# Attention and two expert stages on one core: queries turned once, fillers for TensorE, and value products of two key blocks at a time

## The reference, cut to what matters

```python
# attention: B=4, H=8, S=1152, D=64
q_pool = q.reshape(B, H, S // 2, 2, D).mean(axis=3)      # 576 queries a head
scores = q_pool @ k.T / sqrt(D)
attn = exp(scores - max) ; attn /= attn.sum + 1e-9
x = attn @ v                                             # 2304 rows of 512
# SoLU: x 2304x512, w_in 512x1024, w_out 1024x512
h = x @ w_in ; solu = h * softmax(h)
ln = (solu - mean) / sqrt(var + 1e-6) * g_ln ; x = ln @ w_out
# experts: 8, each 512x1024 and 1024x512, the chosen one times its gate
```

## Time and profile before

| | us |
|---|---|
| median of 3 executions | 1127.13 (1125.83 to 1127.24) |
| the profiled execution | 1129.12 |
| its span, first to last instruction | 1127.4 |
| TensorE busy | 1088.0 (97%) |
| VectorE busy | 750.0 (67%) |
| ScalarE busy | 612.9 (54%) |
| GpSimd busy | 381.5 (34%) |
| mean granted TensorE clock | 0.981 |

### The profile page before, as it was taken

One profiled execution on the slowest core, in us unless ns is written; L12 is line 12 of the kernel. 1 busy time (PEld: TensorE's weight loads), 2 busy tenths in 40 slices (PEclk: granted clock), 3 DMA queues, 4 the chain that ended last, 5 costly groups with the idle time before them and its releaser, 6 DMA issues.

```text
span 1127.4 us, 20403 instructions
## 1 busy us (share of the span) xinstructions
PE 1088.0 (97%) x6647; PEld 767.4 (68%) x6647; DVE 750.0 (67%) x1632; ACT 612.9 (54%) x1327; POOL 381.5 (34%) x454
## 2 busy tenths in 40 slices
PE   7899999999999999999899999997989999999996
PEld 4565665556656565655588888886768888888885
DVE  4777787777778777777548999898775633333110
ACT  5676666667666666665465434435356534343221
POOL 4545544454554445445322211215112211111101
PEclk8899999999999999999899999999999999999998
DMA  4221122212112221102520000004556653311100
GB/s 129 64 60 36 53 64 64 62 47 56 44 48 65 64 64 46 40 21 77 150 85 19 28 20 19 28 30 185 171 180 239 228 182 113 106 38 49 39 21 1
DMA packets 92705, 85.59 MB, mean 76 GB/s; under 512 B 49006, under 2 KB 69486, under 8 KB 92464
## 3 DMA queue, kind: packets, MB, share of 16 engines
q1 hardware_dynamic: 88592, 72.92, 21.0%
q0 software_dynamic: 4000, 11.28, 3.1%
HBM read 74.73 MB, written 11.27 MB: 76 GB/s over the span
## 4 chain that ended last, share of the span: by engine, by line
PE 44%; DVE 2%; issue 2%; POOL 1%; ACT 1%; DMA 1%; DVEq 0%; ACTq 0%; POOLq 0%
PE h_ps L694 8%; PE h_ps L696 8%; PE h_ps L695 8%; PE o_ps L694 5%; PE o_ps L696 5%; PE o_ps L695 5%; PE t_ps L1170 2%; PE t_ps L1062 1%; PE h_ps L1137 1%; PE h_ps L1186 1%; DVE junk L1266 1%; DMA w_raw_e<-in_moe_w 1%; DVE w_split L1480 0%; POOL x_lo L973 0%; PE h_ps L1084 0%
## 5 line engine op out<-in xcount | busy, mean ns | idle before, releaser
L346 POOL TENSOR_SCALAR probs<-probs,scales 128x576 f32<-128x576 f32 x288 | 209.8, 748 | 263.6 <-DVE scales L547 263.6
L642 ACT ACTIVATE probs<-s_ps,lows 128x576 f32<-128x576 f32 x288 | 211.0, 737 | 146.5 <-DVE lows L518 146.1
L518 DVE TENSOR_REDUCE lows<-s_ps 128x1 f32<-128x576 f32 x288 | 205.2, 753 | 59.1 <-PE s_ps L423 51.3
L371 PEld LDWEIGHTS t_ps<-ident,probs 128*128 128x128 f32 x1152 | 123.8, 141 | 108.4 <-issue 100.4
L423 PE MATMUL s_ps<-kt,qt 64*128 64x288 f32 x1024 | 163.9, 438 | 4.8 <-ACT probs L642 4.8
L371 PE MATMUL t_ps<-ident,probs 128*128 128x128 f32 x1152 | 158.8, 281 | 2.8 <-POOL probs L346 2.0
L472 PE MATMUL pv_ps<-pt,values 128*64 128x512 f32 x576 | 155.2, 618 | 1.0 <-DVE x_t L582 1.0
L556 DVE COPY pt<-t_ps 128x512 f32<-128x512 f32 x144 | 99.4, 690 | 43.7 <-PE t_ps L371 43.6
L423 PEld LDWEIGHTS s_ps<-kt,qt 64*128 64x128 f32 x1024 | 89.3, 190 | 43.4 <-issue 24.5
L992 POOL DMA_INDIRECT out<-junk,target_rows x25 | 29.5, 1182 | 261.0 <-ACT junk L1699 260.7
L637 ACT COPY pt<-t_ps 128x512 f32<-128x512 f32 x144 | 84.4, 586 | 28.5 <-PE t_ps L371 24.5
(11 more groups left out here) (257 smaller groups left out, 2056.2 us busy)
## 6 DMA issues: line engine op xcount, KB each, us to landing
w_raw_e<-in_moe_w SPq DMA_DIRECT2D x60, 512.0 KB, 5.5
k_raw<-in_k SPq DMA_DIRECT2D x32, 256.0 KB, 2.8
q_raw<-in_q SPq DMA_DIRECT2D x32, 256.0 KB, 3.2
token_rows<-x_rows SPq DMA_DIRECT2D x18, 256.0 KB, 2.0
values<-in_v SPq DMA_DIRECT2D x32, 128.0 KB, 2.7
values<-in_v SPq DMA_DIRECT2D x64, 64.0 KB, 2.7
w_raw<-in_moe_w_in SPq DMA_DIRECT2D x4, 512.0 KB, 5.0
w_raw<-in_moe_w_out SPq DMA_DIRECT2D x4, 512.0 KB, 3.8
```

What stands on the lines that cost most here:

```text
L346: nc.gpsimd.tensor_scalar(where, where, scales[:, g % 2, s, c:c + 1], 1.0, ALU.mult, ALU.mult).then_inc(norm_done if c else half_scaled, 1)
L371: last = nc.tensor.transpose(bank[:, i * P:(i + 1) * P], source, ident[:])
L518: nc.vector.tensor_reduce(lows[:, g % 2, s, c:c + 1], s_ps[c][:, :, 0:part], AX.XY, ALU.max, negate=True).then_inc(low_done[c], 1)
L642: nc.scalar.activation(two_halves(probs[g % 2][:, s, :])[:, :, columns(c)], s_ps[c][:, :, 0:part], ACT.Exp, bias=lows[:, g % 2, s, c:c + 1 ...
```

## The change

- **Queries turned once.** `q_raw` and `q_sum` hold both heads; GpSimd adds both in one instruction, without writing the sum twice. Four transposes turn them (piece Q, slot 1), ScalarE copies the bank to `qx` (head 0 on partitions 0 to 63, head 1 above), and four DMAs (`move_queries`) copy the halves to both halves of `qt`. Piece QB and its visit in slot 7 are gone. Pair 0 keeps the old way (`FIRST_QA`, `FIRST_QB`). S of slot 0 waits for `q_moved` too.
- **SP's order** in the loop: the keys `load_a(at + 2)` first, then the values, the moves, both query loads, the rest. SoLU's first weights load a pair earlier.
- **First pair.** The next pair's pieces are turned in slots 4 to 7 instead of 0, 1, 2, 6, 7; TensorE gets filler transposes (`warm`) in each slot, four or eight; the warm-up before the data mixes shapes. `merge_scales(0, 2)` comes after the score minimum of slot 8 instead of before it.
- **Drain.** ScalarE splits `w_in` in slots 1, 2, 6, 7 of the last pair, and `w_out` one slot earlier than before; in slot 1 of `at` = 16 the value products stand between the two halves of the turns; eight fillers end the block.
- **SoLU entry.** The first low part is computed by VectorE (`first_x_lo`) instead of GpSimd; twelve fillers stand before `up(0)`.
- **Two blocks at a time.** `multiplied` gives slot 2 the pair's block 0, slot 4 blocks 1 and 2, slot 6 blocks 3 and 4, slot 8 blocks 5 and 6, slot 1 of the next pair blocks 7 and 8. `pt` has three buffers instead of two.

```diff
-    KA, QA, TAILS, KB, QB = range(5)
-    kq_slots = {0: KA, 1: QA, 2: TAILS, 6: KB, 7: QB}
+    KA, Q, TAILS, KB = range(4)
+    FIRST_QA, FIRST_QB = range(4, 6)
+    kq_slots = {0: KA, 1: Q, 2: TAILS, 6: KB}
+    first_kq_slots = {4: KA, 5: Q, 6: TAILS, 7: KB}
...
-        def multiplied_index(at, s):
-
-            i = slots * at + s - slots - 2
-            return i if 0 <= i < key_tiles * pairs else None
+        def multiplied(at, s):
+
+            i, j = divmod(slots * at + s - slots - 1, key_tiles)
+            blocks = [key_tiles * i + b for b in {1: (0,), 3: (1, 2), 5: (3, 4), 7: (5, 6)}.get(j, ())]
+            if j == 0:
+                blocks = [key_tiles * (i - 1) + b for b in (7, 8)]
+            return [b for b in blocks if 0 <= b < key_tiles * pairs]
...
+            def move_queries(n):
+                sp.wait_ge(kq_out, kq_count(n, Q))
+                for h in range(2):
+                    first = h * (full + 1)
+                    for u in range(2):
+                        sp.dma_start(qt[n % 2][rows(u), first:first + full, :].rearrange("p t n -> p (t n)"),
+                                     qx[rows(h), :]).then_inc(q_moved, 16)
...
             for at in range(pairs + 1):
+                n = at + 2
+                if n < pairs:
+                    sp.wait_ge(kq_done, kq_count(n - 1, KA))
+                    load_a(n)
                 if at < pairs:
                     if at >= 2:
                         sp.wait_ge(pv_done, key_tiles * (at - 1))
                     load_values(at)
-                n = at + 2
+                if at + 1 < pairs:
+                    move_queries(at + 1)
                 if n < pairs:
-                    sp.wait_ge(kq_done, kq_count(n - 1, KA))
-                    load_a(n)
-                    sp.wait_ge(q_sums, sum_count(n - 1, QA))
-                    load_qa(n)
+                    sp.wait_ge(q_sums, sum_count(n - 1, Q))
+                    load_q(n, 0)
+                    load_q(n, 1)
...
-            add_queries(0, 1)
-            add_queries(1, 0)
+            add_first_queries()
+            add_queries(1)
             add_tail(1)
             for g in range(pairs):
-                if g + 1 < pairs:
-                    add_queries(g + 1, 1)
                 normalise(g, 0)
                 if g + 2 < pairs:
-                    add_queries(g + 2, 0)
+                    add_queries(g + 2)
                     add_tail(g + 2)
...
-            for i in range(18):
-                nc.tensor.transpose(s_ps[1][:, 1, 0:P], ident[:], ident[:])
...
+            def warm(bank, times):
+                for i in range(times):
+                    nc.tensor.transpose(bank[:, 0:P], ident[:], ident[:])
...
                     if at == 0:
                         score_tile(at, s, at)
...
                         third_visit(at, s, at)
+                        warm(pv_ps, 4 if s < 2 or has_kq(at, s) else 8)
                         continue
                     if i is not None:
                         turn_tiles(i, 0)
+                        if at == pairs and s == 1:
+                            for m in multiplied(at, s):
+                                multiply(m)
                         turn_tiles(i, 1)
                     third_visit(at, s, at)
                     if at < pairs:
                         score_tile(at, s, at)
-                    if m is not None:
-                        multiply(m)
+                    if not (at == pairs and s == 1):
+                        for m in multiplied(at, s):
+                            multiply(m)
...
-                    if s == 8 and at < pairs:
+                    if s == slots - 1 and 0 < at < pairs:
                         merge_scales(at, 2)
...
             def up(m):
-                pe.wait_ge(x_lo_done, m + 1)
+                if m == 0:
+                    pe.wait_ge(first_x_lo, 1)
+                else:
+                    pe.wait_ge(x_lo_done, m)
...
+            for i in range(12):
+                nc.tensor.transpose(o_ps[:, 0:P], ident[:], ident[:])
             for at in range(tiles + 2):
```

More of the change, by code:

```diff
@@ L96, in build_attention @@
         k_tail = in_arena("k_tail", [P, 2, dim])
-        q_raw = [in_arena(f"q_raw{h}", [P, full, 2 * dim]) for h in range(2)]
+        q_raw = in_arena("q_raw", [P, full, 2, 2 * dim])
         q_tail = in_arena("q_tail", [P, 2 * dim])
-        q_sum = [in_arena(f"q_sum{h}", [P, full, 2, dim]) for h in range(2)]
+        q_sum = in_arena("q_sum", [P, full, 2, dim])
+        first_q_sum = in_arena("first_q_sum", [P, full, 2, dim])
+        kt_size = 2 * half
         kt = [in_arena(f"kt{i}", [P, 2, half]) for i in range(2)]
@@ L108, in build_attention @@
         tail_sum = sb("tail_sum", [P, 2, dim])
+        qx = sb("qx", [P, main])
         gains = sb("gains", [P, w_out.shape[0] // P])
-        pt = [sb(f"pt{i}", [P, 2 * main]) for i in range(2)]
+        pt = [sb(f"pt{i}", [P, 2 * main]) for i in range(3)]
         pt_rest = sb("pt_rest", [P, key_tiles, P])
@@ L304, in _ @@
                     load_b(n)
[L305 to L307 removed]
+                if at == pairs - 2:
                     for c in range(stages):
@@ L361, in _ @@
                     normalise(g, b)
+            pool.wait_ge(t_done[1], key_tiles * (pairs - 1))
             for c in range(in_chunks):
@@ L382, in kq_blocks @@
                     return [merged(k_tail[:]), merged(tail_sum[:])]
-                return [merged(q_sum[piece == QB][:, t, :, :]) for t in range(full)]
+                source = first_q_sum if piece == FIRST_QB else q_sum
+                return [merged(source[:, t, :, :]) for t in range(full)]
             def raw_ready(n, piece):
@@ L485, in multiply_rest, with warm_halves, warm_quarters @@
                 last.then_inc(pv_rest_done, 1)
-            for i in range(18):
-                nc.tensor.transpose(s_ps[1][:, 1, 0:P], ident[:], ident[:])
-            for piece, bank in ((KA, t_ps[0]), (QA, t_ps[1]), (TAILS, third_ps)):
+            def warm(bank, times):
+                for i in range(times):
+                    nc.tensor.transpose(bank[:, 0:P], ident[:], ident[:])
+            def warm_halves(times):
+                for i in range(times):
+                    for u in range(2):
+                        nc.tensor.transpose(s_ps[1][:, u, 0:dim], ident[rows(u), :], ident[rows(u), rows(u)])
+            def warm_quarters(times):
+                for i in range(times):
+                    for u in range(2):
+                        for h in range(2):
+                            nc.tensor.matmul(s_ps[1][rows(h), u, 0:dim], ident[rows(u), rows(h)],
+                                             ident[rows(u), rows(u)], start=True, stop=True)
+            warm(pv_ps, 3)
+            warm_halves(8)
+            warm(pv_ps, 2)
+            warm_quarters(4)
+            warm(pv_ps, 4)
+            for piece, bank in ((KA, t_ps[0]), (FIRST_QA, t_ps[1]), (TAILS, third_ps)):
                 raw_ready(0, piece)
@@ L594, in _ @@
                                 merge_lows(at, b)
-                            if s == end and b < 2:
+                            if s == end and (b < 2 or at == 0):
                                 merge_scales(at, b)
@@ L618, in copy_kq @@
                     last = scaled(kt[par][:, int(piece == KB), 0:main], bank[:])
+                elif piece == Q:
+                    last = scaled(qx[:], bank[:])
                 elif piece == TAILS:
@@ L622, in copy_kq @@
                 else:
-                    first = 0 if piece == QA else full + 1
+                    first = 0 if piece == FIRST_QA else full + 1
                     last = scaled(qt[par][:, first:first + full, :].rearrange("p t n -> p (t n)"), bank[:])
```

108 lines of the change are left out of this document (63 added, 45 removed).

## The result

The changed kernel takes 1136.18 us (median of 4 runs, 1135.06 to 1137.33), the kernel before 1126.89 beside it (4 runs). The ratio is 1.0089, 95% interval 1.0071 to 1.0106: slower by 9.3 us.

What follows compares the result with a forecast made beforehand. TensorE, busy 97% of the span, was taken to bound the kernel. Middle +7.8, first pair +3.8, drain 0 and SoLU entry -3.6 gave +8.0 us on the 1127.13 median: 1135, range 1127 to 1141.

Steps and rivals of the forecast that it cites:

- First SoLU matmul 3.6 us closer: SoLU entry: a sign that the forecast is right, the first SoLU matmul coming 3.6 us closer.
- turns of queries: Slot 7 of a pair: one third-bank visit of four turns fewer, 0.44 us less in 14 pairs, -6.2 us.
- merging M: Slots 1, 4, 6, 8: two value products (M) together save 0.06 us, four times a pair, 15 pairs, -3.6 us.
- wait in slot 1 (and 0): Slot 1: second half of the key block's turns waits 0.7 us for GpSimd's normalisation, at fourteen boundaries, +9.8 us.
- wait for exponentials: Short slots: scores wait for ScalarE's exponentials, 0.42 us from slot 7 to 8, 0.10 from 3 to 4, +7.8 us.
- first pair: First pair: late query loads and GpSimd's sums of pair 2 delay normalisation and next turns, +3.8 us, +1.5 to +5.
- drain: End of attention: 30.1 us from the last scores to the last value product, as before: 0, +-0.7 us.
- SoLU entry and all behind it: SoLU entry: -1.2 us from VectorE's first low part, -2.4 from fillers holding the clock over 12 matmuls, together -3.6.
- S to T: Scores followed straight by turns: taken like scores to value product, bounds +-0.09, +-5.4 us; upper-bound rival 1140, chance 0.08.
- The fillers hold no clock: Rival, SoLU entry and first pair: filler transposes don't hold the clock, +2.4 and about +1.5 us, 1139; chance 0.12.
- GpSimd not held in the first pair: Rival, first pair: loads land before normalisation is due, next turns at 37.4, -9.6 us, 1125.5; chance 0.12.
- The wait in slot 1 does not come: Rival, slot 1: the merge's chain is 0.7 us shorter, so no wait, -9.8 us, 1125.3; chance 0.06.

Runs made afterwards that it cites:

- single products: The changed kernel with the value product of one block in every slot again, three buffers kept: 1129.24 us, ratio to the kernel before 1.0016.
- The run with the early copy: Changed kernel, one value product per slot, GpSimd's pair 2 sums after first pair's normalisation, ScalarE's rest copy to x_t in slot 8: 1116.14 and 1115.05 us.
- product pairs alone: The kernel before with only the pairs of value products and the third buffer of pt: 1142.16 us, ratio 1.0131.
- the run with GpSimd's order: The changed kernel with GpSimd's sums of pair 2 placed after the first pair's normalisation batches: 1129.99 us, ratio 1.0028.

## Why the prediction was right, and where its terms were off

The sign, the time (1135 against 1136.2) and the mechanism came out, and what it said to look for is there: GpSimd's late batch and TensorE waiting for it, the waits in slots 1 and 8, a pair of 33.3. Two statements in it were wrong without harm to the sum. "First SoLU matmul 3.6 us closer": the matmul is 1.0 closer, and the rest is the speed of those behind it, as in its own sum. And the 30.1 us of the drain "from the last S to the last M" are in no row: it is 28.07 before and 27.39 after. Its sum, term by term, against the two traces:

| term | predicted | in the traces |
|---|---|---|
| turns of queries | -6.2 | -6.0 |
| merging M | -3.6 | -8.5 |
| wait in slot 1 (and 0) | +9.8 | +9.8 |
| wait for exponentials | +7.8 | +11.3 |
| first pair | +3.8 | +4.9 |
| drain | 0 | 0 |
| SoLU entry and all behind it | -3.6 | -3.7 |
| sum | +8.0 | +7.8 |

The first four are the per-pair figures times 14 (0.43, 0.61, 0.70, 0.81). They add to 6.6; the stretch from S of slot 4 in the second pair to that of the last is longer by 6.8, and with it the sum is the 8.0 of the spans. That this equals the forecast is in part luck: two terms were off by 4.9 and 3.5 us, on opposite sides, and the times of the runs differ by 9.3.

- *Merging M* was the worst-sized term. I read 0.06 from the one place where two M stand together, the end of attention (2.03 against 1.08), and those are modelled ends. In the steady state two M to T take 1.87 against 2.02. The same row in the changed kernel shows 1.94. A saving that comes four times a pair needed a bound from both sides, which I gave only to S to T. That one came out at 1.17 to 1.18, the value taken.
- *Waits for the exponentials*: the place was right (slots 4 and 8), the size was 0.53 and 0.20 instead of 0.42 and 0.10, and slot 6 isn't quite free (0.08). S of slot 8 starts 2.49 after S of slot 7, the 2.48 of the earlier trace rows, and the M behind it 1.41 later, 3.90 in all; the forecast amounts to 3.78. The 0.1 that I had allowed for the semaphore and the first load in slot 1, and not here, would be of that size; that it is this was not shown.
- *The wait in slot 1* was sized at 0.70, and that is what it is in 11 of 13 pairs. GpSimd starts 2.24 and ends 3.71 after T of slot 0, as in the kernel before. Where slot 0 loses 0.20, slot 1 loses 0.50: GpSimd's end sets when the second half of T starts, so a wait ahead of it is a part of the same 0.70. That it came through the merge is shown by the run that moves the merge.
- *Queries turned once* is a term that holds only beside the others. With product pairs it is worth 33.68 - 33.25 = 0.43 a pair. With single ones it is worth 32.79 - 32.77, nothing: slot 8 comes 0.44 sooner, and the copy to x_t behind VectorE's work isn't sooner. The prediction said that ScalarE loses a copy and is idle anyway, and did not ask what is late next. In the change slot 0 waits for that copy only in two of 13 pairs, since its slot 8 is longer (5.63 from T to T, 4.25 with single products), and there the wait lies under the one for GpSimd. The run with the early copy shows what single products lost: 32.38.
- *First pair*: every step was there, 1 to 1.5 us later each. GpSimd's long batch starts at 35.36 (33.8 predicted) and ends at 44.02 (42.5), next T at 48.20 (46.9). SP issues the two query loads at 28.23 (28.3), so the delay is in the landing (the sum starts at 32.51, 32.0 predicted) and most of all in the last sum, which waits for its own load (1.16). The fillers did what was claimed: S of slot 4 at 18.04 (17.9), of slot 8 at 28.02 (27.8).
- *Drain*: 41.15 against 41.18. It is a zero of two parts. The product pairs alone make it 2.8 longer, with 1.60 of waiting for GpSimd between the halves of T. With everything but the product pairs it is 39.0, 2.2 shorter than before. The prediction had both parts as nothing. What in the rest of the change brings the 2.2 was not tried apart; the brackets of TensorE's rows show 1.18 for GpSimd, 1.04 for x_t and 0.85 for copies of T before, and 0.18, 0.58 and 0.24 with single products in the changed kernel, where an M stands between the halves of T.
- *SoLU entry*: -1.02 by the earlier first matmul (-1.2 predicted) and the 12 slow matmuls gone. In the run without them the fillers are worth 1.3, as only 8 are slow there. The 2.4 holds against the profiled execution of before; product pairs alone, with the same entry, had 8 too.

The rivals. *The fillers hold no clock* fell: the windows show 1.00 against 0.73. The Trainium skill, "TensorE: Matmul & The Clock Gate", Part 4: PE-mode transpose, says that full clock does not engage for transposes. By these rows turns of 128x128 in f32 did hold it here, beside the scores in the first pair and by themselves at the entry. The rival's price for the first pair (+1.5) is what the traces have up to the wait for GpSimd (1.5). *GpSimd not held in the first pair* is what the run with GpSimd's order makes true: 1130 and not 1125.5. The next T comes at 40.33 and not at 37.4, as the third visit then waits for the sum and the clock falls in the wait for T; that is 2.9 of the 4.5, and 1.2 is what the change itself lay above the forecast. *The wait in slot 1 does not come* fell, and S to T did not cost its upper bound.

Between the two theories of the experiments, both have their part: 6.9 us for the product pairs and 6.2 for the order of GpSimd's queue, each tried by itself, and the sum of all that is repaired, from 1136.2 to 1115 or 1116, has 4.5 to 5.5 more for the copy (4.8 in the middle by the traces). The change's other parts, with GpSimd's order and the copy repaired, are a gain of 11 to 12.5 us over the kernel before.

## What to carry to other kernels

When work that stands once in each slot is put into every second one, the bound engine's total falls, and short slots run into loops between the other engines: compare each short slot with the length of those loops, not the mean slot. An operation with an old operand that is queued behind one with a fresh operand is late for no reason of its own: look for it wherever a slot gets shorter, for it eats the saving. In a prologue, count what stands ahead of each queue's urgent work, SP's and GpSimd's alike.

## What the runs showed that I had not expected

- Two of VectorE's smallest operations change their length without a change of their own. In slot 7 the low and below took 0.16 and 0.59 us before, 0.50 and 0.68 with single products. Before:

```profile
294.13 0.16 DVE L527 TENSOR_TENSOR low<-lows 128x2 f32<-128x2 f32 x1
```

  and with single products:

```profile
299.69 0.50 DVE L580 TENSOR_TENSOR low<-lows 128x2 f32<-128x2 f32 x1
```

  Together with the start of the next it is 0.42 us, the very time by which the minima of slot 8, the operation on below and the copy to x_t are later, counted from S (below ends 4.07 after S of slot 8, 3.64 before). GpSimd is at work in both cases, so that doesn't tell them apart. The cause was not tried.
- Turns keep TensorE's granted clock at 1.00: 4 or 8 of them in each slot of the first pair, beside the scores (0.73 from 20 to 30 us without them), and 20 of them by themselves ahead of SoLU.
- In stretches whose code was the same, the low clock lasted differently long from one run's trace to another: 3.4 or 6.8 us behind the wait in the first pair, 6.8 or 10.2 us ahead of the experts. A difference of 1 to 2 us between two profiled executions can be this alone.
- Two value products in a row save 0.15 us over two apart, with the same matmuls.
